# Windowed attention, MLP and routed experts on one core: a reordered load queue and an earlier score step in the attention prologue

## The reference

```python
# 1. attention with a causal window of 128 and a linear bias per head
scores = q @ k.T / sqrt(64) + slope[h] * (-|i - j|), masked to 0 <= i - j < 128
attn_out = softmax(scores) @ v                      # x: (2304, 512)
# 2. gated MLP, w_in (512, 2048), w_out (2048, 512)
h = x @ w_in
x = (h * clip(h + 3, 0, 6) / 6) @ w_out
# 3. eight experts, one for each token, w1 (8, 512, 1024), w2 (8, 1024, 512)
expert = argmax(cosine(x, expert_emb) / tau)
out = gate * (relu(x @ w1[expert]) @ w2[expert])
```

## Time and profile before

| what | value |
|---|---|
| median of three runs | 851.38 us |
| the profiled execution's own time | 850.99 us |
| its span, first to last instruction | 849.3 us |
| mean granted TensorE clock | 0.986 of full speed |
| TensorE busy (matmuls) | 828.0 us, 97% of the span |
| VectorE / ScalarE / GpSimd busy | 56% / 47% / 29% |
| DMA | 80.20 MB, mean 94 GB/s |

### The profile page before, as it was taken

How to read it: one execution, slowest core, us unless ns; L and a number is a source line. 1 busy time by engine, 2 the same in 40 slices (tenths; PEclk the granted TensorE clock), 3 DMA queues, 4 the chain that set the end, 5 groups by cost and what they waited for, 6 DMA issues and landing times.

```text
span 849.3 us, 18688 instructions
## 1 busy us (share of the span) xinstructions
PE 828.0 (97%) x6508; PEld 709.7 (84%) x6508; DVE 478.0 (56%) x1469; ACT 396.1 (47%) x1056; POOL 242.6 (29%) x262
## 2 busy tenths in 40 slices
PE   6979999999999999999999999999999999999996
PEld 4868888888888888888888888878888888888885
DVE  7645577665676666766666578766554434554000
ACT  4655555554545555455454336534343434333342
POOL 5991000000000000000000101277666556666432
PEclk8898999999999999999999999999999999999999
DMA  8662411111112112111110006474455544442100
GB/s 239 209 175 73 141 51 46 56 39 38 51 51 67 35 50 64 52 50 33 33 39 1 27 25 192 158 260 149 151 160 169 160 137 139 151 150 81 43 19 11
DMA packets 54428, 80.20 MB, mean 94 GB/s; under 512 B 11752, under 2 KB 28136, under 8 KB 54210
## 3 DMA queue, kind: packets, MB, share of 16 engines
q1 hardware_dynamic: 50050, 67.58, 25.9%
q0 software_dynamic: 4000, 11.29, 4.1%
q10 hardware_dynamic: 288, 0.13, 0.1%
HBM read 69.51 MB, written 11.30 MB: 95 GB/s over the span
## 4 chain that ended last, share of the span: by engine, by line
PE 88%; POOL 5%; DMA 3%; DVE 2%; SPq 1%; issue 1%; ACT 0%; POOLq 0%; ACTq 0%; DVEq 0%
PE ps_h L833 22%; PE ps_y L850 20%; PE ps_h L973 16%; PE ps_s L1012 15%; PE ps_out L778 3%; PE ps_s L741 3%; PE ps_y L997 3%; POOL wout_lo L571 2%; POOL win_lo L571 2%; PE ps_out L1012 1%; DMA y_scratch<-gate_tok 1%; PE ps_out L937 1%; PE ps_s L760 1%; PE ps_s L766 1%; DMA en_all<-in_moe_w_out 1%
## 5 line engine op out<-in xcount | busy, mean ns | idle before, releaser
L833 PE MATMUL ps_h<-x_hi,win_hi 128*128 128x256 f32 x576 | 166.7, 297 | 0.0
L833 PE MATMUL ps_h<-x_lo,win_hi 128*128 128x256 f32 x576 | 159.0, 284 | 0.0
L833 PE MATMUL ps_h<-x_hi,win_lo 128*128 128x256 f32 x576 | 159.0, 284 | 0.0
L1118 ACT CAST gated_hi<-gated 128x256 fp32r<-128x256 f32 x144 | 58.4, 406 | 137.4 <-PE ps_y L850 99.6
L1381 DVE TENSOR_TENSOR gated_lo<-gated,gated_hi 128x256 fp32r<-128x256 f32 x144 | 64.4, 447 | 102.6 <-ACT gated_hi L1118 102.6
L833 PEld LDWEIGHTS ps_h<-x_hi,win_hi 128*128 128x128 f32 x576 | 108.7, 192 | 8.3 <-issue 3.2
L612 POOL MEMSET arena<- 128x64 bf16 x2 | 0.2, 152 | 400.5 <-DVE x_lo L1355 400.5
L850 PE MATMUL ps_y<-wout_hi,gated_hi 128*128 128x512 f32 x288 | 114.0, 396 | 0.0
L850 PE MATMUL ps_y<-wout_hi,gated_lo 128*128 128x512 f32 x288 | 113.8, 395 | 0.0
L850 PE MATMUL ps_y<-wout_lo,gated_hi 128*128 128x512 f32 x288 | 112.1, 389 | 0.0
L833 PEld LDWEIGHTS ps_h<-x_hi,win_lo 128*128 128x128 f32 x576 | 108.7, 192 | 2.3
(11 more groups left out here) (232 smaller groups left out, 1566.3 us busy)
## 6 DMA issues: line engine op xcount, KB each, us to landing
arena<-in_moe_w SPq DMA_DIRECT2D x64, 512.0 KB
arena<-in_v SPq DMA_DIRECT2D x40, 128.0 KB, 3.1
y_scratch<-y_sb SPq DMA_DIRECT2D x9, 512.0 KB, 3.8
en_all<-in_moe_w_in SPq DMA_DIRECT2D x16, 256.0 KB, 4.1
arena<-in_v SPq DMA_DIRECT2D x16, 256.0 KB, 3.1
en_all<-in_moe_w_out SPq DMA_DIRECT2D x16, 256.0 KB, 3.3
arena<-in_q SPq DMA_DIRECT2D x31, 128.0 KB, 2.4
arena<-in_k SPq DMA_DIRECT2D x31, 128.0 KB, 2.9
```

The costliest lines, as they stand in the source:

```text
L833: last = pe.matmul(ps_h[m % 2][:, 0:TB], a[:, c, w], r[:, c, x], start=n == 0, stop=n == 3 * KC - 1)
L1118: act.copy(gh[m % 2][:], gate[:]).then_inc(act_gh, 1)
```

## The change

Four edits, three of them to SP's queue, one to TensorE's order.

1. `load_qk(4)` is issued in the prologue, right behind piece 0 and `load_v(0)`, so ahead of pieces 1 to 3 and `load_v(1)`; it was at it = 1.
2. `scores(4)` is done at it = 2, behind `values(0)`; it was at it = 3, behind `values(1)` and `transposes(2)`.
3. Pieces are asked for four ahead in SP's order instead of six: at it = 5 pieces 12 to 15 come first instead of 12 to 17, and slot m asks for pieces 12 + 2m + 4 and the next. There are still six places, and the wait of each fetch is unchanged.
4. `load_v(g)` from g = 3 on is issued one iteration sooner: at it = 2g - 1 instead of 2g.

```diff
                 if n == 0:
                     load_v(0)
+                    load_qk(4)
             load_v(1)
             for it in range(LASTK + 1):
-                if 0 < it < STEPS - 3:
+                if 1 < it < STEPS - 3:
                     load_qk(it + 3)
...
                 if it == FIRST:
-                    for n in range(AHEAD_OF[it], ALONE + WR):
+                    for n in range(AHEAD_OF[it], ALONE + 4):
                         fetch_w(n)
...
                 for m in slots(it):
                     for n in split_by_act(m):
-                        if n + WR < W_PIECES:
-                            fetch_w(n + WR)
-                            fetch_w(n + WR + 1)
+
+                        if n + 4 < W_PIECES:
+                            fetch_w(n + 4)
+                            fetch_w(n + 5)
...
                 for g in range(3, NG):
-
-                    if NQ * (g - 1) + OUT == it:
+                    if NQ * (g - 1) - 1 + OUT == it:
                         load_v(g)
...
                 if it == 2:
                     values(0)
-                if it == 3:
                     scores(4)
```

## The result

The changed kernel takes 842.87 us (median of 6 runs, 842.18 to 844.2) beside 851.38 us (median of 6, 850.6 to 852.83) of the kernel before: ratio 0.9901, interval 0.9887 to 0.9914. That is 8.5 us. The forecast was 843.6 us with a range of 840.8 to 846.0. The profiled execution took 842.24 us with a span of 840.5 us, 8.8 us less than the span of before.

What follows compares the result with a forecast made beforehand. TensorE was taken as the bound, busy 828.0 us of a 849.3 us span, with gains possible only ahead of 90 us. 4.42 + 2.58 + 0.75 = 7.75 us gave a median of 843.6 us, range 840.8 to 846.0 us.

Steps and rivals of the forecast that it cites:

- Part 1: At `values(6)`: values issued from about 41.2 us, so PE's wait for v goes, 4.42 us gained; four-ahead order priced at nothing.
- Part 2: Values, scores and `up(10)` behind that wait run at full clock, 3.10 instead of 5.68 us: 2.58 us gained.
- With no idle stretch ahead there is nothing to lower the clock: At `values(6)` to `up(10)`: without the wait ahead the clock stays at full, worth 2.58 us.
- Part 3: At the start: step 4 loaded and scored earlier, first `up` at 24.8 instead of 26.28 us, 0.75 us gained after clock loss.
- the term for the clock: At the first `up`: clock rises at 27.6 us as before, so 0.75 of the 1.5 us gained is lost.
- rival A: At the start: clock rises sooner, giving back another 1.4 to 3 us, 840.6 to 842.2 us; chance 0.20.
- PE asks for pieces with over 1.5 us in hand, so nothing: At the start: POOL some 0.6 us later from piece 4 on costs PE nothing.
- What was to be late next: ScalarE ahead of `up(12)`: table loads beside PE's work leave 1.9 us in hand; loss taken as nothing, 1 us at most.
- B: ScalarE or the place of piece 22, 24 or 30 holds PE, or the start gives nothing: 844.6 to 846.6 us; chance 0.19.
- C: At `values(6)`: something besides the values also ends the wait, leaving 2 to 4 us and cold clock: 847 to 849.5; chance 0.05.
- E: The change does nothing, as waits for places move `load_v(3)` as late as before: 851.4 us; chance 0.02.
- D: At the start: late step 4 loads make `scores(4)` hold `values(1)` and all behind: slower, 853 to 855 us; chance 0.04.

Runs made afterwards that it cites:

- experiment 1: Kernel before with only the values of groups 3 and up asked for one iteration sooner: 845.19 us, ratio 0.9919.
- experiment 3: Changed kernel without the start's two edits, so pieces four ahead and values a step sooner only: 843.41 us, ratio 0.9905 against the kernel before.
- Experiment 2: Kernel before with only the pieces asked for four ahead, values where they were: 848.03 us, ratio 0.9959.
- experiment 4: Kernel before with only the start's two edits, loads and scores of step 4 moved up: 851.69 us, ratio 1.0002.
- experiment 9: Changed kernel with ten idle-filling matmuls on TensorE around the transposes of step 2: 843.51 us, ratio 0.9905 against the kernel before.
- experiment 10: Changed kernel with the values of group 1 asked for ahead of pieces 1 to 3: 845.65 us, ratio 0.9941 against the kernel before.
- experiment 11: As experiment 10, with ScalarE also making the high parts of pieces 4 and 5: 843.92 us, ratio 0.9923 against the kernel before.
- experiment 6: Changed kernel with scores of step 4 back at it = 3, its loads still early: 843.45 us, ratio 0.9899 against the kernel before.
- experiment 8: Changed kernel with piece 1 ahead of step 4's loads and ScalarE making high parts of pieces 4 and 5: 842.63 us, ratio 0.9896 against before.

## Why the prediction was right, and where it was off

**Part 1, the wait.** Right: the 4.42 us are gone. The values were issued 0.7 us later than worked out (41.91 us, not 41.2), since POOL was 0.76 us late where 0.6 was said. I priced the four-ahead order at nothing; the profiles of experiments 1 and 3 give it a worth: 0.73 us ahead of `values(6)` and 0.5 us at `up(12)`. For pieces 22 and 24 I had feared up to 1 us of loss in the changed kernel; it is the kernel without the four-ahead order that loses time there.

**Part 2, the clock behind it.** 2.48 us against 2.58. Experiment 2 bears the mechanism out: a wait of 1.46 us left the clock up. The estimate by the Trainium skill for the same stretch, 2.84 us (TensorE: Matmul & The Clock Gate, Terms), lies on the same side and further off. "With no idle stretch ahead there is nothing to lower the clock" held for this stretch and not in general: at 485 us in experiment 3 the clock fell with 0.5 us of PE idle in the 20 us around it.

**Part 3, the start.** The landings and starts held: `scores(4)` at 12.65 (13.0), `values(2)` at 18.57 (18.2), the first `up` at 24.92 (24.8), POOL 0.74 us late at piece 1 (0.9). What failed is the term for the clock: "If it rises at 27.6 us as before". It rose at 25.7 us, so 1.63 us came through instead of 0.75. The profiled execution was forecast at 843.2 us and took 842.24, and 0.88 of these 0.96 us are this term. For the median, 0.7 us under its forecast, the same cause is likely but no trace shows its clock. That is rival A in part. The chain of waits shows what bounds the start now, the last transfer of group 1's values:

```profile
11.30 7.22 DMA arena<-in_v
```

The Trainium skill's fit for a transfer (DMA: Bandwidth & Descriptors, Anatomy of one DMA), as an estimate, gives 2.3 us for this one of 128 KB and 2.6 us for the first of the three, of 256 KB; the trace has 7.22 us in this crowd, so it was right not to use it.

"PE asks for pieces with over 1.5 us in hand, so nothing" failed as a general statement. It held in the first profile of the changed kernel (1.7 us in hand at `up(4)`); in experiments 4, 9, 10 and 11 PE comes to `up(4)` ahead of POOL's piece 11, in 4 and 9 because the clock rose early, in 10 and 11 because the values of group 1 came ahead of the pieces too. The start's edits do bring PE forward. `up(3)` begins at 35.09 us before, at 33.53 and 33.17 us in the changed kernel's two profiles, and at 31.5 and 32.3 us in experiments 4 and 6; without these edits it begins at 34.01 us in experiment 1, whose clock rose early, and at 35.3 and 35.7 us in experiments 3 and 2. How much of that reaches the end depends on POOL and ScalarE behind it. The worth in the medians, 0.5 us between experiment 3 and the changed kernel, is not clear of the spread. By the medians the queue's edits gave 8.0 us instead of 7.0 and the start's 0.5 instead of 0.75; the split into parts rests on the rows of the profiles, the sum on the times.

**What was to be late next.** ScalarE's timeline of the changed kernel, beside the earlier trace rows:

```profile
48.70 0.62 ACT L1150 CAST wout_hi<-en_all 128x512 fp32r<-128x512 f32 x1 [1.53 <-DMA en_all<-in_moe_w_out]
50.48 0.62 ACT L1150 CAST win_hi<-en_all 128x512 fp32r<-128x512 f32 x1 [1.16 <-DMA en_all<-in_moe_w_in]
...
58.92 1.28 ACT L1220 ACT_TABLE_LOAD   x1
...
61.21 1.28 ACT L1079 ACT_TABLE_LOAD   x1
...
63.40 0.46 ACT L1114 ACTIVATE clip<-ps_h,half 128x256 f32<-128x256 f32 x1
```

The table loads moved beside PE's work as said. From the first load to the clip's start are 4.5 us; `up(12)` began at 64.65 us without a wait, with its gate some 0.3 us ahead of it. I had 1.9 us in hand, which was too much by 1.6: ScalarE began the first load 2.25 us behind the start of `values(6)`, where the prediction has 0.5 us. The timeline suggests why: from piece 24 on ScalarE never idles over half a microsecond until the gate of slot 9, so its waits for pieces 22 and 24 are carried along; no experiment took them away alone. In experiments 1, 8 and 9 the hand was gone and PE lost 0.5 to 0.7 us at `up(12)`. Each load is 1.28 us with the next operation close behind. The Trainium skill (ScalarE: Activation LUTs, What ACT_TABLE_LOAD costs) has 2.66 us for a switch with its drain; by that, as an estimate, PE would have waited some 2.4 us, which no row shows.

**The rivals.** A happened in part. B's waits of ScalarE for pieces 22 and 24 are there, 1.53 and 1.16 us, and reach PE in none of the rows of the changed kernel's first profile; in its second a `down` waits 0.26 us for its gate, and in experiments 1, 8 and 9 `up(12)` waits as B has it. C and E fall with the missing wait. (C was added up wrong: 2 to 4 us of wait and 2.6 us of clock on top of 843.6 us are 848.2 to 850.2 us, not 847 to 849.5.) D was built: 846.86 us, so it costs 4 us and not the sign.

## What to carry to other kernels

In an in-order queue of loads a late transfer is to be looked for in what stands ahead of it and what that waits for: here four weight pieces, each held for a place, made a load of 3.6 us come 4.4 us late. A short idle stretch of TensorE costs its length and, if the clock falls with it, what the work behind it takes longer until the clock is back: count both (4.42 and 2.48 us here, 2.99 and 1.6 us in experiment 10, 1.46 us and nothing in experiment 2). And time gained ahead of an event that another engine paces is worth nothing until that pace is moved (851.69 us for the start's edits alone).

## What was not expected of the hardware

The point at which TensorE's clock comes up for good at the start differs between executions, even of the same program: 25.7 us in the first profile of the changed kernel, 22.3 us in the second. The granted clock in the records is no guide there: in experiment 1 it reads 1.00 from the start, as the stretch from 15 us shows,

```profile
15.00:16.00 1.00, 0.18 (x9) 0.01 (x1) 1.00 (x7) 0.34 (x2) 0.92 (x2) 1.00 1.08 219
```

while its timeline has the same pair of transposes at two speeds:

```profile
9.31 0.66 PE L760 MATMUL ps_h<-ident,arena 128*128 128x128 f32 x2 [0.18 <-DVE arena L1337]
...
21.63 0.38 PE L763 MATMUL ps_h<-ident,arena 128*128 128x128 f32 x2
```

So until the first change is recorded, the durations tell the clock and the column doesn't. In that execution the full clock came near 21 us, in the first profile of the changed kernel near 25.7, in that of before near 27.6. No run here shows what sets the point; the fillers of experiment 9 did not settle it.

The second surprise is far behind the change. In four of the thirteen profiles (experiments 1, 3, 4 and 6) the clock falls once more between 484 and 498 us, for 3.4 us, and costs 1.3 to 1.5 us. PE's idle time in the stretch from 480 to 500 us is 0.5 us in experiments 1, 3 and 6, and the same in the profiles of before and of the changed kernel, where the clock stays up. What sets it off isn't shown. The two together fit the spread of 1 to 5 us among runs of one kernel, and they are why a single profiled execution can't be set against a median: differences under about 2 us have to be read from PE's rows ahead of 480 us, or from many runs.
